# The first pair of an attention kernel: its first load in two halves by head, its scores and maxima head by head

## The chip, the cores and the metric

The kernel runs on one core of a Trainium2 chip. The metric is the device time of one execution in microseconds (us), the median of the runs. TensorE (PE, with its weight loads PEld) multiplies matrices, VectorE (DVE), ScalarE (ACT) and GpSimd (POOL) work on elements, and SyncE (SP) issues transfers. Each engine has its own queue of instructions, taken in order; semaphores order the queues among each other.

## The reference

A block of causal attention with a linear memory, followed by two feed-forward networks, all in float32. 4 batches of 8 heads, 576 positions, 64 values per head:

```python
def _attn_ref(q, k, v, M_prev, z_prev, beta):
    scores = scale * np.matmul(q, k.transpose(0, 1, 3, 2))
    scores = np.where(causal, -1000000000.0, scores)
    scores = scores - scores.max(-1, keepdims=True)
    a = np.exp(scores)
    a /= a.sum(-1, keepdims=True) + 1e-09
    local = np.matmul(a, v)
    q_p = phi(q)                    # phi(x) = max(x, 0) + min(exp(x), 1)
    mem_ret = np.einsum('bhsd,bhde->bhse', q_p, M_prev)
    mem_norm = np.einsum('bhsd,bhd->bhs', q_p, z_prev)[..., None] + 1e-06
    mem_out = mem_ret / mem_norm
    g = 1.0 / (1.0 + np.exp(-beta))[None, :, None, None]
    return g * mem_out + (1 - g) * local
def reference(...):
    x = attention output as 2304 tokens x 512
    x = _moe_ref(x)     # (silu(x @ w_gate) * (x @ w_val)) @ w_out, inner width 1536
    return _moe2_ref(x) # g(x @ w_in) @ w_out with a clipped square g, inner width 2048
```

## The kernel before, in words

The 32 heads are taken two at a time, as 16 pairs. In a pair the 576 rows of queries are cut into tiles: i = 4, 3, 2, 1 of 128 rows each, in this order, and the first 64 rows. Tile i needs width(i) = 64 + 128 i columns of keys because of the causal mask: 576, 448, 320 and 192. In the numbering of the kernel j = 4 p + k is tile 4 - k of pair p, so j = 0 is tile 4 of pair 0, j = 1 its tile 3.

For every tile TensorE makes the scores of both heads (`scores`, line 1390; head 0 lies on partitions 0 to 63 of `qk`, head 1 on 64 to 127, and each writes its own columns of PSUM), VectorE adds the mask, negates, takes the row's extreme and writes `negs` and `nmax` (`tile_max`, line 1067, head by head, each with a readout), ScalarE takes the exponential and its sum (`exp_tile`, 807), VectorE makes the factor of the memory part from that sum and the norms (`mem_scale`, 1086), GpSimd writes the memory's rows beside the exponentials (`mem_rows`, 681), TensorE turns both over (`turn`, 1420), ScalarE and VectorE copy them from PSUM (`copy_pt`, 828 and 1105), and TensorE multiplies with V and the memory (`values`, 1442 and 1447). The scores of the first 64 rows are one product (`scores_f`, 1400).

The norms of a pair go another way. ScalarE takes exp(q) (`exp_q`, 797), GpSimd max(q, 0) (`relu_q`, 654), VectorE joins them (`phi`, 1041), GpSimd multiplies with z in two instructions (`phi_z`, 662 and 664, which write `qz`), VectorE sums (`norm_q`, 1047) and takes the reciprocal with the gate (`rnorm_q`, 1052 and 1055); only then can it make the first `mem_scale` of the pair. GpSimd also scales V by the other gate (`v_scale`, 672).

The start, in the order of each queue. SyncE: the columns of `qk` that tile 4 needs, 704 of 1280, as one transfer of 352 KB (line 579, semaphore `ld_first`), the rows `nat` of pair 0, the rest of `qk`, then `nat` of pair 1, V, and so on. ScalarE: a transfer of `beta`, its exponentials (864), `exp_q(0)`, then for pair 0 `exp_tile(0)`, `exp_q(1)`, the wait for `gone` and two copies of it into `cf` (880, 881), `exp_tile(1)` and the rest. GpSimd: masks, `relu_q(0)`, `phi_z(0)`, then `relu_q(1)`, `mem_rows(0)`. VectorE: the small mask, the gates (1137 to 1144) as soon as ScalarE has the exponentials of beta, `tile_max(0)`, a memset and the reciprocal `gone` (1147, 1148), `phi(0)`, `tile_max(1)`, and then the loop: `norm_q(0)`, `rnorm_q(0)`, `mem_scale(0)`, `tile_max(2)`, `tile_max(3)`, and so on. TensorE: 10 idle products of 128x128 on zeros (`idle_products`, 1366; a product of float32 leaves two records in the trace), the scores of tile 4, 4 idle products, `scores_f(0)`, the scores of tiles 3, 2, 1, 8 idle products, and the first `turn`. `scores_f` and the scores of tile 3 both wait until both maxima of tile 4 have been read out (`maxed` at 2), since they write over their columns: tile 3's head 0 and head 1 take the first two banks, which head 0 of tile 4 held.

After the attention of all pairs the two feed-forward networks run on TensorE (lines 1476 to 1478), each product as three on parts of the numbers.

## Time and profile before

| | before |
|---|---|
| median of 3 runs | 979.85 us (979.78 to 980.0) |
| profiled execution, its own time | 979.51 us |
| its span in the trace | 977.70 us |
| PE busy | 966.3 us (99%) |
| DVE, ACT, POOL busy | 696.6, 463.3, 336.2 us |
| attention, until the first feed-forward product | about 183 us of the span |

The profile counts a TensorE record as busy from its start to a modelled end, so records overlap. "Idle before" in brackets is the time for which the engine had nothing to do ahead of a group, with what ended it. A chain of waits follows the last instruction back to what released it, each time to the instruction that came last. Transfers are timed from issue to landing, and a transfer's landing is counted on 16 engines; the median of them is printed.

### The profile page before, as it was taken

Reading aid. Unit: us, or ns where it says so; the run is one execution under the profiler, and the core shown is the slowest. Engines: PE = TensorE matmul, PEld = TensorE weight load, DVE = VectorE, ACT = ScalarE, POOL = GpSimd, SP = SyncE. Lnnn points to the kernel's source line nnn. Section 1 sums busy time; section 2 is a strip of 40 time slices with the busy share of each in tenths; the row PEclk is TensorE's granted clock in tenths of the full one; section 3 lists DMA queues with packets and bytes.
Section 4 is the critical chain, followed back from the end, with each engine's and each line's share of the span. In section 5 each row is a group of like instructions: output and inputs, shape, how many; then the busy total and the mean of one; then the engine's idle time right before and its main releaser. Section 6 shows DMA issues by size and latency. Waiting matters only on the chain.

```text
span 977.7 us, 18964 instructions
## 1 busy us (share of the span) xinstructions
PE 966.3 (99%) x6372; PEld 926.6 (95%) x6372; DVE 696.6 (71%) x1369; ACT 463.3 (47%) x940; POOL 336.2 (34%) x385
## 2 busy tenths in 40 slices
PE   8999999999999999999999999999999999999998
PEld 7777777899999999999999999999999999999998
DVE  6888989576667555557555568888887677867766
ACT  6899999555445222224222246445543333433331
POOL 5777786196782000100000157688410010000000
PEclk9999999999999999999999999999999999999999
DMA  6544543598777755555554544667785744538321
GB/s 246 170 153 155 160 157 110 199 341 286 288 271 307 246 194 199 220 219 217 219 208 194 195 148 169 229 256 258 297 270 200 275 181 174 216 140 301 139 105 65
DMA packets 46157, 204.73 MB, mean 209 GB/s; under 512 B 5488, under 2 KB 5872, under 8 KB 46064
## 3 DMA queue, kind: packets, MB, share of 16 engines
q1 hardware_dynamic: 45920, 203.52, 57.3%
q8 instruction: 54, 0.88, 0.4%
q14 instruction: 39, 0.32, 0.1%
q10 hardware_dynamic: 144, 0.00, 0.0%
HBM read 147.33 MB, written 56.17 MB: 208 GB/s over the span
## 4 chain that ended last, share of the span: by engine, by line
PE 90%; ACT 4%; issue 2%; POOL 2%; DVE 2%; ACTq 0%; DVEq 0%; POOLq 0%
PE ps L1476 26%; PE ps L1478 25%; PE ps L1477 25%; PE ps L1447 5%; PE ps L1390 5%; ACT pt L828 3%; PE ps L1420 3%; POOL wu_l L704 1%; DVE xt_l L1128 0%; PE ps L1366 0%; DVE negs L1067 0%; ACT xt_h L859 0%; ACT rown L807 0%; PE ps L1400 0%; POOL wu_r L689 0%
## 5 line engine op out<-in xcount | busy, mean ns | idle before, releaser
L1476 PE MATMUL ps<-xt_h,wu_h 128*128 128x384 f32 x840 | 281.3, 335 | 0.5 <-DVE wu_l L1119 0.2
L1478 PE MATMUL ps<-xt_h,wu_l 128*128 128x384 f32 x840 | 280.7, 334 | 0.0
L1477 PE MATMUL ps<-xt_l,wu_h 128*128 128x384 f32 x840 | 280.6, 334 | 0.0
L1476 PE MATMUL ps<-hid_h,wd_h 128*128 128x384 f32 x672 | 225.1, 335 | 1.8 <-DVE xy L1240 0.9
L1478 PE MATMUL ps<-hid_h,wd_l 128*128 128x384 f32 x672 | 224.5, 334 | 0.0
L1477 PE MATMUL ps<-hid_l,wd_h 128*128 128x384 f32 x672 | 224.5, 334 | 0.0
L1243 DVE TENSOR_TENSOR xy<-xy,ps 128x384 f32<-128x384 f32 x288 | 158.2, 550 | 69.1 <-PE ps L1478 68.9
L923 ACT ACTIVATE hid_h<-hid_r 128x768 fp32r<-128x768 f32 x84 | 70.8, 842 | 204.9 <-DVE hid_r L1217 140.8
L1476 PEld LDWEIGHTS ps<-xt_h,wu_h 128*128 128x128 f32 x840 | 157.7, 188 | 2.6 <-issue 0.8
L1477 PEld LDWEIGHTS ps<-xt_l,wu_h 128*128 128x128 f32 x840 | 157.7, 188 | 0.0
L1478 PEld LDWEIGHTS ps<-xt_h,wu_l 128*128 128x128 f32 x840 | 157.7, 188 | 0.0
L1476 PEld LDWEIGHTS ps<-hid_h,wd_h 128*128 128x128 f32 x672 | 126.1, 188 | 3.7 <-DVE hid_l L1221 2.3
L1477 PEld LDWEIGHTS ps<-hid_l,wd_h 128*128 128x128 f32 x672 | 126.2, 188 | 0.0
L1478 PEld LDWEIGHTS ps<-hid_h,wd_l 128*128 128x128 f32 x672 | 126.2, 188 | 0.0
L1221 DVE TENSOR_TENSOR hid_l<-hid_r,hid_h 128x768 fp32r<-128x768 f32 x84 | 87.3, 1039 | 40.7 <-ACT hid_h L923 40.6
L739 POOL TENSOR_TENSOR traw<-xy 128x384 f32<-128x384 f32 x20 | 23.1, 1178 | 239.3 <-PE ps L1478 239.3
L807 ACT ACTIVATE rown<-negs,nmax 128x576 f32<-128x576 f32 (+3 forms) x128 | 77.1, 605 | 12.0 <-DVE nmax L1067 11.9
L704 POOL TENSOR_TENSOR wu_l<-wu_r,wu_h 128x256 fp32r<-128x256 f32 x65 | 55.2, 877 | 59.9 <-ACT wu_h L838 59.8
L908 ACT ACTIVATE u2s<-ps 128x384 f32<-128x384 f32 x60 | 29.5, 491 | 96.5 <-PE ps L1478 96.4
L1198 DVE TENSOR_TENSOR hb<-u2s,ps 128x384 f32<-128x384 f32 x60 | 33.1, 551 | 52.9 <-PE ps L1478 52.9
L1227 DVE SCALAR_TENSOR_TENSOR tmp<-tmp 128x768 f32<-128x768 f32 x48 | 52.2, 1089 | 22.9 <-ACT tmp L938 22.6
L938 ACT ACTIVATE tmp<-hb,nhalf 128x768 f32<-128x768 f32 x48 | 45.1, 939 | 48.3 <-DVE hb L1198 34.5
(87 smaller groups left out, 1321.0 us busy)
## 6 DMA issues: line engine op xcount, KB each, us to landing
wu_l<-kept_ul SPq DMA_DIRECT2D x40, 896.0 KB, 7.5
wu_h<-kept_uh SPq DMA_DIRECT2D x40, 896.0 KB, 5.6
kept_uh<-wu_h SPq DMA_DIRECT2D x20, 896.0 KB, 6.0
kept_ul<-wu_l SPq DMA_DIRECT2D x20, 896.0 KB, 6.9
wd_h<-kept_dh SPq DMA_DIRECT2D x28, 512.0 KB, 3.7
wd_l<-kept_dl SPq DMA_DIRECT2D x28, 512.0 KB, 5.2
wu_r<-w_up SPq DMA_DIRECT2D x20, 512.0 KB, 5.2
qk<-qk_in SPq DMA_DIRECT2D x15, 640.0 KB, 5.2
```

Source lines behind the costliest of these rows:

```text
L704: low = nc.gpsimd.tensor_tensor(wu_l[u % 3][:, k], wu_r[u % 3][:, k], wu_h[u % 2][:, k - 1].bitcast(F32), ALU.subtract)
L807: nc.scalar.activation(head_rows(j)[:, h + (i == 1), D:D + w], negs[:, t % NEGS, 0:w], ACT.Exp, bias=nmax[:, p % 2, k:k + 1], scale=-1.0, ...
L923: nc.scalar.activation(hid_h[:, t % 6], hid_r[:, t % 6], ACT.Copy).then_inc(hh_done, 1)
L938: nc.scalar.activation(tmp[:, r], hb[:, u % 2, r], ACT.Relu, bias=nhalf[:], scale=0.5).then_inc(relued, 1)
L1221: nc.vector.tensor_tensor(hid_l[:, t % 6], hid_r[:, t % 6], hid_h[:, t % 6].bitcast(F32), ALU.subtract).then_inc(hl_done, 1)
L1227: nc.vector.scalar_tensor_tensor(tmp[:, r], tmp[:, r], 1.0, tmp[:, r], ALU.min, ALU.mult).then_inc(s_done, 1)
L1243: nc.vector.tensor_tensor(y, y, o, ALU.add).then_inc(evac, 1)
L1390: mm = nc.tensor.matmul(psf[:, col + a0:col + a1], qk[rows, s, P + q0(i):P + q0(i) + P], qk[rows, s, P + S + a0:P + S + a1], start=True, s ...
L1447: mm = nc.tensor.matmul(ps[D * h:D * h + D, bank, col:col + P], vm[:, s, h, c], pt[:, j % PTS, n], start=(c == 0), stop=(c == i))
L1476: nc.tensor.matmul(dst, w_hi, v_hi, start=start, stop=False, skip_group_check=onto)
L1477: nc.tensor.matmul(dst, w_hi, v_lo, start=False, stop=False, skip_group_check=onto)
L1478: return nc.tensor.matmul(dst, w_lo, v_hi, start=False, stop=stop, skip_group_check=onto)
```

## The change

The first load is issued as two transfers, head 0's 64 partitions on SyncE's queue and head 1's on ScalarE's, ahead of `beta`'s, each with a semaphore of its own. Tile 4 of pair 0 has a function of its own, `scores_first`: it waits for head 0's half, issues both products of head 0, waits for head 1's half, issues those of head 1, and signals each head by itself (`scored_first`, `scored`); `tile_max(0)` waits for the one and then the other. `scores_f` and the scores of tile 3 wait for one maximum of tile 4 and not for two, in every pair (in every pair since that wait is written once for all; tiles 2 and 1 still wait for two). On VectorE `tile_max(0)`, `tile_max(1)` and `phi(0)` come right behind the small mask, in this order, and the gates, the memset and `gone` behind them. On ScalarE `exp_tile(1)` comes ahead of the two copies of `gone`. The idle products of the start go from 10, 4 and 8 to 7, none and 12.

```diff
@@ SyncE
-            sp.dma_start(qk[:, 0, cut:], qk_in[0][:, cut:]).then_inc(ld_first, 16)
+            sp.dma_start(qk[0:D, 0, cut:], qk_in[0][0:D, cut:]).then_inc(ld_first[0], 16)
@@ ScalarE
+            cut = P + q0(SLOTS)
+            act.dma_start(qk[D:P, 0, cut:], qk_in[0][D:P, cut:]).then_inc(ld_first[1], 16)
             act.dma_start(betas[:, 0], beta.rearrange("(o h) -> o h", o=1).broadcast_to([P, 2 * HPB])).then_inc(ld_beta, 16)
...
+                if p < NPAIR:
+                    exp_tile(j + 1)
                 if p == 0:
                     act.wait_ge(gone_set, 1)
...
                 if p < NPAIR:
-                    exp_tile(j + 1)
                     exp_tile(j + 2)
@@ VectorE
-                at_least(dve, scored, j + 2 if i == 2 else j + 1)
+                if j > 0:
+                    at_least(dve, scored, j + 2 if i == 2 else j + 1)
                 for h in range(2):
                     t, k = 2 * j + h, block_of(i, h)
+                    if j == 0:
+                        dve.wait_ge((scored_first, scored)[h], 1)
...
             nc.vector.tensor_copy(maskf[D:P], mask[D:P, S - D:S]).then_inc(maskf_set, 1)
+            dve.wait_ge(maskf_set, 2)
+            tile_max(0)
+            tile_max(1)
+            phi(0)
             dve.wait_ge(gexp_e, 2)
...
-            dve.wait_ge(maskf_set, 2)
-            tile_max(0)
             nc.vector.memset(cf[0:D, :, 0], 1.0).then_inc(cf_set, 1)
             nc.vector.reciprocal(gone[:], gexp[:, 1]).then_inc(gone_set, 1)
-            phi(0)
-            tile_max(1)
@@ TensorE
-            idle_products(10)
+            idle_products(7)
...
-                if j == 0:
-                    pe.wait_ge(ld_first, 16)
-                else:
+                if j > 0:
                     at_least(pe, ld_qk[s], 16 * (p // 2 + 1))
...
-                    at_least(pe, maxed, 2 * SLOTS * p + 2)
+                    at_least(pe, maxed, 2 * SLOTS * p + (1 if i == 3 else 2))
...
+            def scores_first():
+
+                i, w = SLOTS, width(SLOTS)
+                for h in range(2):
+                    rows = slice(D * h, D * h + D)
+                    col = score_col(i, h)
+                    pe.wait_ge(ld_first[h], 16)
+                    for a0, a1 in ((0, 512), (512, w)):
+                        mm = nc.tensor.matmul(psf[:, col + a0:col + a1], qk[rows, 0, P + q0(i):P + q0(i) + P],
+                                              qk[rows, 0, P + S + a0:P + S + a1], start=True, stop=True)
+                    mm.then_inc((scored_first, scored)[h], 1)
...
             def scores_f(p):
...
-                at_least(pe, maxed, 2 * SLOTS * p + 2)
+                at_least(pe, maxed, 2 * SLOTS * p + 1)
...
-                if p < NPAIR:
+                if p == 0:
+                    scores_first()
+                elif p < NPAIR:
                     scores(SLOTS * p)
...
-                if p == 0:
-                    idle_products(4)
...
                     if p == 0:
-                        idle_products(8)
+                        idle_products(12)
                     turn(SLOTS * p, (0, 1))
```

## Rows read from the trace of the kernel before

**Rows 1.** The page, part 4: engines' shares of the chain

```profile
...
PE 90%; ACT 4%; issue 2%; POOL 2%; DVE 2%; ACTq 0%; DVEq 0%; POOLq 0%
...
```

**Rows 2.** Chain of waits in order: start us, length us, what

```profile
...
5.67 1.75 PE ps L1390 x8
...
9.15 0.41 PE ps L1400 x2
...
11.74 0.68 DVE norm L1047
...
18.60 1.23 POOL vm L672
...
19.87 1.31 PE ps L1447 x20
...
30.63 1.28 PE ps L1447 x20
...
```

**Rows 3.** DMA issues before 1 us: count, KB each, us to landing

```profile
...
qk<-qk_in SPq DMA_DIRECT2D x1, 352.0 KB, 4.8
...
```

**Rows 4.** Stretches: busy by engine, granted clock, DMA share, GB/s

```profile
...
2.00:5.00 3.00, 3.00 (x16) 3.00 (x15) 0.45 (x2) 0.44 (x1) 0.21 (x1) 1.00 0.60 135
...
```

**Rows 5.** Weight loads: lines of 2:5 and 11.35:13, timeline of 5.6:6.7

```profile
...
L1366 PEld LDWEIGHTS ps<-pt 128*128 128x128 f32 x15 | 3.3, 333 | 0.0
...
L1366 PEld LDWEIGHTS ps<-pt 128*128 128x128 f32 x16 | 1.9, 191 | 0.2 <-issue 0.2
...
5.62 0.53 PEld L1390 LDWEIGHTS ps<-qk 64*128 64x128 f32 x4 [0.24 <-issue]
6.64 0.20 PEld L1390 LDWEIGHTS ps<-qk 64*128 64x128 f32 x2 [0.49 <-issue]
```

**Rows 6.** Timeline of TensorE: start, length, what, [idle before]

```profile
...
1.03 4.64 PE L1366 MATMUL ps<-pt 128*128 128x128 f32 x20 [1.03 <-DVE pt L1132]
...
7.34 1.16 PE L1366 MATMUL ps<-pt 128*128 128x128 f32 x8
...
9.49 1.89 PE L1390 MATMUL ps<-qk 64*128 64x448 f32 x12
...
14.93 1.30 PE L1390 MATMUL ps<-qk 64*128 64x512 f32 x8
...
```

**Rows 7.** Timeline of VectorE, same columns

```profile
...
6.11 0.19 DVE L1137 TENSOR_SCALAR gexp<-gexp 128x64 f32<-128x64 f32 x1 [3.63 <-ACT gexp L864]
...
7.56 0.76 DVE L1067 CUSTOM_DVE_ANT_0 negs<-ps,mask 128x576 f32<-128x576 f32 x1 [0.70 <-PE ps L1390]
8.25 0.08 DVE L1067 DVE_READ_ACCUMULATOR2_ANT nmax<- 128x1 f32 x1
...
8.93 0.08 DVE L1067 DVE_READ_ACCUMULATOR2_ANT nmax<- 128x1 f32 x1
8.96 0.32 DVE L1148 RECIPROCAL gone<-gexp 128x32 f32<-128x32 f32 x1
...
9.20 0.69 DVE L1041 SCALAR_TENSOR_TENSOR qp<-qexp,qrelu 128x576 f32<-128x576 f32 x1
10.56 0.62 DVE L1067 CUSTOM_DVE_ANT_0 negs<-ps,mask 128x448 f32<-128x448 f32 x1 [0.67 <-PE ps L1390]
...
11.66 0.75 DVE L1047 TENSOR_REDUCE norm<-qz 128x9 f32<-128x576 f32 x1
...
```

**Rows 8.** Timeline of GpSimd, same columns

```profile
...
9.98 0.32 POOL L662 TENSOR_TENSOR qz<-qp,nat 128x64 f32<-128x64 f32 x1 [1.27 <-DVE qp L1041]
10.25 1.28 POOL L664 TENSOR_TENSOR qz<-qp,nat 128x512 f32<-128x512 f32 x1
...
```

**Rows 9.** Timeline of ScalarE, same columns

```profile
...
9.99 0.68 ACT L797 ACTIVATE qexp<-nat 128x576 f32<-128x576 f32 x1
...
11.23 0.67 ACT L807 ACTIVATE rown<-negs,nmax 128x448 f32<-128x448 f32 x1
...
13.71 0.56 ACT L807 ACTIVATE rown<-negs,nmax 128x320 f32<-128x320 f32 x1 [1.07 <-DVE nmax L1067]
...
```

More of the change, by code:

```diff
@@ L153, in attention_two_ffns @@
         r_in = [sem(f"r_in{s}") for s in range(2)]
-        ld_first = sem("ld_first")
+        ld_first = [sem(f"ld_first{h}") for h in range(2)]
+        scored_first = sem("scored_first")
         r_row = sem("r_row")
```

## The prediction

> **What bounds the kernel now.** I read four views. First the page: the chain that ended last is TensorE for nine tenths of the span [rows 1], so almost everywhere the time is set by a queue that the change doesn't touch. Then the chain in order of time, from the start to the second pair [rows 2]. It shows where the change can act: the first scores (ending at 5.67 + 1.75 = 7.42 us), the first maxima, the rest of pair 0's scores from 9.15, VectorE's sum of the norms at 11.74, GpSimd's scaling of V at 18.60, and TensorE's first products with V at 19.87. The same products of the next pair come at 30.63, 10.76 us later, and from 19.87 on the attention part of the chain is TensorE's queue with ScalarE's copies between its pieces, pair after pair. So the first 19.87 us are a lead-in, and whatever it gains or loses is, by this chain, handed to the end one for one. Third, the transfers and TensorE's early rows [rows 3 to 6], which say what sets the first score. Fourth, the engines' timelines from 6 to 14 us [rows 7 to 9], which say how long each step of the lead-in takes and who is waiting.
>
> **The first load.** Today one transfer of 352 KB lands at a median of 4.8 us after its issue at 0.72 [rows 3], that is about 5.5, and the weight load of the first scores starts at 5.62 [rows 5]. The 10 idle products (20 records) fill TensorE from 1.03 to 5.67 [rows 6]. Between 2 and 5 us the DMA engines move only 135 GB/s [rows 4]. The change gives each head 176 KB on its own queue. Bounds for head 0's start S: below, the 7 idle products that are left, 1.03 + 14/20 x 4.64 = 4.28; above, today's 5.65, should the halves share the engines so evenly that the first comes with the last. In the row's terms the 352 KB at 135 GB/s are 2.7 us and half of them 1.3, but the other half runs beside it and the next transfer moves up behind it. I take S = 4.8, nearer to today, for that reason, and head 1 some tenths later; since the two heads use different halves of the array, head 1 overlaps with head 0 as now.
> On this point the Trainium skill (DMA: Bandwidth & Descriptors, Rules for kernel authors) speaks against the change: transfers to two partition halves, from one queue or two, serialize on the same 16 engines and are better left as one. No row of before has two such halves. By that rule S stays at 5.65 and the shift below would be +1.78 (rival B).
>
> **The clock.** The page prints a granted clock of 1.00 from the start, but the rows say otherwise: the weight loads of the idle products take 333 ns each between 2 and 5 us and 191 ns after 11 us [rows 5], the lower and the upper of TensorE's two levels. The first scores straddle the rise: first passes at 5.62 to 5.65, second passes at 6.64 (0.99 us later, with weight loads that are short again) [rows 5], all done at 7.42, so 0.78 after 6.64. A tile of the same shape wholly at the upper level takes 1.30 us [rows 6]. A pass over 512 columns streams as long as four idle records of 128: by the busy time of the weight loads beside them, 4 x 3.3/15 = 0.88 us at the lower level and 4 x 1.9/16 = 0.48 at the upper [rows 5]. If the clock rises when it did, near 6.6, scores that start at 4.8 run: first passes to 5.79, second passes at the lower level to 6.67, and the short rest, 0.78 - 0.48 = 0.30, to about 7.0. So 0.85 us of earlier start buy only 0.42 us: the first maximum starts at 7.14 and not at 7.56 [rows 7].
>
> **From the first maximum to the norms, before and after.** Before: VectorE takes the maxima of both heads of the first tile (7.56, the second read out at 8.93 + 0.08 = 9.01), then runs the reciprocal and phi(0) (9.20, 0.69) while TensorE computes the scores of tile 3, waits 0.67 us for these, takes tile 3's maxima from 10.56, and starts the sum over qz at 11.66 [rows 7]. GpSimd's two products for it ran from 9.98 to 10.25 + 1.28 = 11.53 [rows 8], just hidden by tile 3's maxima. From first maximum to that sum: 11.66 - 7.56 = 4.10 us.
> After: TensorE waits for head 0 alone. Head 0's maximum is read out at 8.25 + 0.08 = 8.33, 0.77 after its start [rows 7]. From a readout to the first-rows product 9.15 - 9.01 = 0.14 [rows 2, 7], from there to tile 3's scores 9.49 - 9.15 = 0.34 [rows 2, 6], from there to tile 3's maxima 10.56 - 9.49 = 1.07: 2.32 us from the first maximum, where VectorE has been free since 9.01 - 7.56 = 1.45. Tile 3's maxima then take 11.66 - 10.56 = 1.10. Only then comes phi(0), which used to lie in the gap: 0.69, then 0.09 to GpSimd, 1.55 for its two products, 0.13 back: **2.32 + 1.10 + 0.69 + 0.09 + 1.55 + 0.13 = 5.88 us, against 4.10: 1.78 us longer.** The 0.87 us gap (2.32 - 1.45) in front of tile 3's maxima is now empty, and the wait for GpSimd behind phi is new. This is the main term: tile 3's maxima come earlier by 0.68 on this clock, but nothing in the chain wants them, while phi(0) is wanted by GpSimd and moves from 9.20 to about 10.6 + 0.1.
> Everything else I cost at nothing, with its cover. The gate block on VectorE (from 6.11 to 7.56 - 0.70 = 6.86, and the reciprocal, 0.32 with a memset beside it [rows 7]: 1.1 us) moves into the new 1.77 us wait for GpSimd; uncovered it would cost 1.1. ScalarE now has exp_q(1) waiting for phi(0), with the exponentials of tile 3 queued behind it, then the two gate copies: from phi's end at 11.26, 0.1 + 0.68 [rows 9], then tile 3's exponentials, today from 11.23 to the start of the idling at 13.71 - 1.07 = 12.64 (1.4), then the gate copies, today between 9.99 + 0.68 and 11.23 (0.6), so about 14.1. The next thing wanted of it is tile 2's exponential, which today starts at 13.71 after 1.07 us of idling [rows 9] and will be wanted at 15.1. About 1 us of cover is left. The load of beta issues one descriptor set later; its users now run four microseconds later. The loads of pair 2 wait for qz and go out later by the shift; their use is a period later than the 14.93 at which pair 1's scores start [rows 6], near 25.6, and a landing took 4.8 us. In the later pairs the softer wait (one maximum for two) changes nothing that the chain shows: there the turns of the pair before stand between tile 4's scores and this wait, and VectorE has 2% of the chain [rows 1]. The idle products moved behind the scores (12 instead of 8) end before the first turn as now, since that waits for GpSimd's row.
>
> **Sum.** Advance of the first maximum -0.42, longer way +1.78: **+1.36 us** at the sum over qz, and from there every engine's order is the same as before, so TensorE's products at 19.87 go to 21.2 and the end with them. The profiled execution takes 979.51 us (span 977.70); it becomes 980.87. The median of the runs lies 0.34 above the profiled one, so 979.85 + 1.36 = 981.2 us.
>
> **Rivals.**
> *A, the clock rises late (slower).* Three idle products fewer leave TensorE empty from 4.28 to 4.8, and the four behind the first scores, which today run from 7.34 for 1.16 us [rows 6], are gone, leaving it empty from about 7.0 to 8.05. If by this the rise comes only after about 8 us, the first scores end at about 7.15 (the 0.30 grows to some 0.5), and the product of first rows and tile 3's scores, 1.39 us, run at the lower level and grow by about 1.0. Shift: -0.28 + 1.78 + 1.0 = +2.5, 982.4; if the first turn is still slow, some 0.8 more, 983.2. For it: today's rise followed 5.6 us of unbroken products. Against: it rose within the first tile, and most of the stretch before stays filled.
> *B, the halves land together.* S = 5.65, no advance: +1.78, 981.6; with head 0 0.3 later still, 982.0. For it: one set of engines at 135 GB/s. Against: nothing runs there before, so that the low rate may be a start-up that two queues pass sooner. This is the case that the rule of the Trainium skill (same page and section) describes.
> *C, early clock.* S = 4.28 and the whole tile at the upper level, 1.30: first maximum at 5.72, an advance of 1.84, against 1.78: nothing gained or lost, 979.8. A rise about 1 us earlier than now gives +0.4 to +0.9. This is also the most that the change can give by its own means.
> *D, the delay is absorbed.* If V's scaling were late for another reason than the norms, the way would not count and only the advance would: 979.4. Against: the chain goes through the sum of norms at 11.74 and GpSimd at 18.60 [rows 2].
>
> **How the numbers follow.** Main case 0.56 (its own range +1.06, S = 4.28 with a late rest, to +1.78: 980.9 to 981.6), A 0.20, B 0.12, C 0.07, D 0.05. The range leaves out D, the lower half of C and the upper part of A: 980.1 to 982.9. A measurement of this kernel can tell about 0.2% from no change, 1.96 us; the line lies at 981.81. Slower: A, four tenths of B, a little of the main case: 0.27. Faster by 0.2% needs an advance that even C doesn't give: 0.01. Same: 0.72.
>
> **What would show it.** After the change: the first weight load of the scores near 4.9, the next pass at 6.6; tile 3's maxima on VectorE near 9.5 with idle time before them released by the scores; phi near 10.6; GpSimd's first qz product near 11.4; the sum over qz near 13.0 with idle time released by GpSimd; first products with V near 21.2, next ones 10.76 later. The prediction is wrong if the sum over qz starts before 12.3 (the first scores came much earlier, or at the upper level), or if weight loads after 7 us still take 333 ns (A), or if the interval from first maximum to the sum isn't near 5.9.

## The result and the profile after

The changed kernel takes 983.67 us (median of 7 runs, 982.37 to 984.49) against 980.00 us for the kernel before beside it (7 runs, 979.77 to 980.74): a ratio of 1.0037, with an interval of 1.0028 to 1.0047. It is slower, by about 3.7 us where 1.4 were forecast, and lies 0.8 us above the range. The profiled execution is the second longest of the seven. The profiled execution took 984.36 us with a span of 982.5 (before: 979.51 and 977.7), so the two traces are 4.8 us apart.

The chain's shares are those of [rows 1] but for a point of VectorE:

```profile
PE 90%; ACT 4%; issue 2%; POOL 2%; DVE 1%; DMA 1%; SPq 0%; ACTq 0%; DVEq 0%; POOLq 0%
```

The new item is DMA with 1%: the chain of the changed kernel begins with a transfer. Its steps in order of time (start, length, what):

```profile
1.97 5.41 DMA qk<-qk_in
...
7.43 0.58 PE ps L1419 x2
8.01 1.82 PE ps L1396 x4
...
11.03 0.67 DVE qp L1046
...
12.18 1.18 DVE gt L1156
...
13.40 0.60 DVE gt L1156
...
14.56 0.62 DVE norm L1052
...
16.60 1.06 PE ps L1439 x8
...
17.70 2.32 PE ps L1396 x8
...
23.71 1.24 PE ps L1466 x20
...
34.40 1.28 PE ps L1466 x20
```

Against [rows 2], the sum of the norms is at 14.56 instead of 11.74 and the first products with V at 23.71 (23.64 in TensorE's timeline) instead of 19.87. The next ones start 10.73 us later in both timelines (at 34.37; before at 30.60). From there the distance between the two traces stays at 3.7 to 3.8 us as far as 640 us: the lead-in hands its delay on one for one, as forecast. A last 0.95 us is added near 650 us (see the end).

The starts in the lead-in, from the timelines of both traces:

| start of, us | before | after | later by |
|---|---|---|---|
| first scores | 5.65 | 4.27 | -1.38 |
| first maximum | 7.56 | 5.72 | -1.84 |
| product of first rows | 9.15 | 7.43 | -1.72 |
| tile 3's maxima | 10.56 | 9.85 | -0.71 |
| phi(0) | 9.20 | 10.94 | +1.74 |
| GpSimd's product for qz ends | 11.53 | 13.33 | +1.80 |
| sum over qz | 11.66 | 14.47 | +2.81 |
| first turn (TensorE) | 13.83 | 16.60 | +2.77 |
| first products with V | 19.87 | 23.64 | +3.77 |

Three engines' timelines tell where it goes (start, length, engine, line, operation, out<-in, count, [idle before and what ended it]). TensorE:

```profile
4.27 2.19 PE L1409 MATMUL ps<-qk 64*128 64x512 f32 x8
7.43 0.58 PE L1419 MATMUL ps<-qk 128*128 128x64 f32 x2 [0.96 <-DMA qk<-qk_in]
7.93 3.38 PE L1396 MATMUL ps<-qk 64*128 64x448 f32 x12
...
16.60 1.06 PE L1439 MATMUL ps<-ident,rown 128*128 128x128 f32 x8 [2.40 <-POOL rown L683]
17.70 2.32 PE L1396 MATMUL ps<-qk 64*128 64x512 f32 x8
```

VectorE:

```profile
9.85 0.62 DVE L1075 CUSTOM_DVE_ANT_0 negs<-ps,mask 128x448 f32<-128x448 f32 x1 [2.58 <-PE ps L1396]
...
10.94 0.76 DVE L1046 SCALAR_TENSOR_TENSOR qp<-qexp,qrelu 128x576 f32<-128x576 f32 x1
...
12.11 1.89 DVE L1156 COPY gt<-gexp 64x16 f32<-64x16 f32 x2
...
14.47 0.70 DVE L1052 TENSOR_REDUCE norm<-qz 128x9 f32<-128x576 f32 x1
```

GpSimd:

```profile
12.06 1.27 POOL L666 TENSOR_TENSOR qz<-qp,nat 128x512 f32<-128x512 f32 x1
13.30 1.64 POOL L656 TENSOR_SCALAR qrelu<-nat 128x576 f32<-128x576 f32 x1
```

The reader is to see five things. Head 0 is scored early. TensorE then stands empty for 0.96 us, until the product of first rows is released by the transfer of the rest of the first pair's q and k. Tile 3's scores take 3.38 us against 1.89 in [rows 6], with 1.92 instead of 1.07 until their maxima can start. Two copies of 64x16 elements take 1.89 us. And the tile after the first turn takes 2.32 us against the 1.30 of [rows 6]. The granted clock says why the scores are slow (stretch; per engine in the order PE, PEld, DVE, ACT, POOL its busy time; clock, where 1.00 is the upper of TensorE's two levels, 2.4 GHz, and 0.50 the lower, 1.2 GHz; DMA share; GB/s):

```profile
7.60:9.50 1.90, 1.90 (x6) 1.06 (x8) 0.00 (x0) 1.11 (x4) 0.03 (x1) 0.50 1.04 423
9.50:11.00 1.50, 1.50 (x10) 1.02 (x6) 1.15 (x5) 0.00 (x0) 0.00 (x0) 0.50 0.78 314
14.00:17.80 3.80, 1.35 (x12) 0.98 (x11) 3.37 (x18) 1.89 (x7) 1.44 (x3) 1.00 0.91 321
17.80:21.20 3.40, 3.40 (x14) 2.38 (x15) 2.99 (x9) 1.95 (x8) 2.97 (x5) 0.50 1.00 407
```

The clock was at its upper level from 4.3 us (the weight loads change from 333 to 190 ns there), fell to the lower one from 7.6 to 11.0, and fell again from 17.8 to 21.2. Ahead of the first fall TensorE was empty from 6.46 to 7.43, ahead of the second for 2.40 us.

Not every execution had both falls. This one has a mean granted clock of 0.997 over its span. Five of the other six have 0.998, as have the traced executions of e4, g1 and g3, each with one fall of 3.1 to 3.5 us, and the last (984.49 us) has 1.0. So in most executions of the changed kernel one fall is likely, and by f1 and g4 below it is the one at the first turn; the first fall, 1.0 us in the split that follows, belongs to this trace.

**The 2.81 us at the sum over qz, split by these rows:** first maximum -1.84; the longer way, as forecast, +1.78; wait for the rest of q and k +0.81 (7.43, where head 0's readout at 6.48 plus the usual 0.14 gives 6.62); lower clock on the product of first rows (0.50 to tile 3's scores, not 0.34) +0.16 and on tile 3's scores (1.92, not 1.07) +0.85; phi to the end of qz +0.06; the gate block +1.01 (14.47 - 13.33 = 1.14 from the end of qz to the sum, where the forecast has 0.13). The parts add up to 2.83. The slow tile of the second pair adds the next 1.0 behind the sum.

### The profile page after: what moved, and what is told of

The parts are those of the page before. It is cut to its first block, busy times and chain, and to the rows that moved or that the text cites. A ratio compares the mean times of both kernels' runs of the same rounds, so it can differ in the third digit from the quotient of the medians.

```text
span 982.5 us, 18953 instructions
## 1 busy us (share of the span) xinstructions
PE 968.9 (99%) x6366; PEld 927.5 (94%) x6366; DVE 698.0 (71%) x1369; ACT 462.9 (47%) x940; POOL 335.3 (34%) x385
## 4 chain that ended last, share of the span: by engine, by line
PE 90%; ACT 4%; issue 2%; POOL 2%; DVE 1%; DMA 1%; SPq 0%; ACTq 0%; DVEq 0%; POOLq 0%
PE ps L1495 26%; PE ps L1496 25%; PE ps L1497 25%; PE ps L1466 5%; PE ps L1396 5%; PE ps L1439 3%; ACT pt L830 3%; DMA qk<-qk_in 1%; POOL wu_l L706 1%; PE ps L1419 0%; ACT wu_h L840 0%; ACT rown L809 0%; POOL wu_r L691 0%; POOL wu_r L689 0%; DVE xy L1251 0%
## 5 line engine op out<-in xcount | busy, mean ns | idle before, releaser
L1075 DVE CUSTOM_DVE_ANT_0 negs<-ps,mask 128x576 f32<-128x576 f32 (+3 forms) x128 | 63.7, 553 | 10.2 <-PE ps L1396 6.9
```

The source lines that it names most:

```text
L1075: nc.vector.tensor_tensor_reduce(negs[:, t % NEGS, 0:w], psf[:, col:col + w], mask[:, S - w:S], -(float(D) ** -0.5), 3.0e38, ALU.add, ALU. ...
```

## The experiments

Fifteen kernels ran, in four groups on one chip each. "Trace" is how much later than before (19.87 us) the first products with V start in the one profiled execution; "median" is the difference of the medians to the kernel before in the same group. The ratio is taken over all executions and is not the quotient of the medians.

| kernel | median us | less before | ratio, 95% interval | trace |
|---|---|---|---|---|
| e1_fill | 983.68 | +4.31 | 1.0049 (1.0030 to 1.0067) | +2.13 |
| e2_phi | 980.84 | +1.47 | 1.0012 (1.0003 to 1.0021) | +0.43 |
| e3_fill_phi | 980.21 | +0.84 | 1.0009 (1.0000 to 1.0019) | +1.74 |
| e4_gates | 981.90 | +2.53 | 1.0025 (1.0015 to 1.0034) | +2.73 |
| f1_order | 984.65 | +5.00 | 1.0049 (1.0034 to 1.0064) | +5.21 |
| f2_load | 982.20 | +2.55 | 1.0025 (1.0015 to 1.0034) | +1.97 |
| f3_idle | 983.19 | +3.54 | 1.0031 (1.0020 to 1.0042) | +3.00 |
| f4_before | 979.37 | -0.28 | 1.0001 (0.9991 to 1.0010) | -0.32 |
| g1_own_idle | 983.69 | +4.32 | 1.0046 (1.0029 to 1.0063) | +3.33 |
| g2_first_7 | 980.26 | +0.89 | 1.0009 (1.0000 to 1.0019) | +0.58 |
| g3_no_middle | 981.02 | +1.65 | 1.0015 (1.0006 to 1.0025) | +1.95 |
| g4_order_fill | 982.81 | +3.44 | 1.0038 (1.0023 to 1.0053) | +2.92 |
| h1_halves | 981.46 | +1.79 | 1.0014 (1.0005 to 1.0023) | -0.01 |
| h2_soft_phi | 980.03 | +0.36 | 1.0001 (0.9992 to 1.0010) | -0.36 |
| h3_best | 979.45 | -0.22 | 1.0000 (0.9991 to 1.0009) | -0.42 |

Trace and median need not agree to better than about 1 us, since the moments at which the clock rises and falls differ from one execution to the next; two rows, e1 and h1, are further apart and are taken up below.

**The changed kernel with its clock held.** The four idle products stand ahead of `scores_f`, as before.

```diff
+                if p == 0:
+                    idle_products(4)
...
-                        idle_products(12)
+                        idle_products(24)
```

> The changed kernel with TensorE kept busy in its two holes: 4 idle products behind the first scores, and 24 instead of 12 before the first turn. Theory (three causes: phi behind tile 3's maxima; the clock falls in the holes; the gate copies and GpSimd's products slow each other): weight loads stay near 190 ns from the rise on, the scores of pair 1's tile 4 take 1.3 us and not 2.3, tile 3's maxima start about 8.9 and not 9.85, the sum over qz starts near 13.5 and not 14.5, first products with V near 21.8 (1.9 later than before), time about 981.9 us. Rival (the clock is all of it): about 980 us, like before. Rival (the clock plays no part): unchanged, 983.7 us.

Measured: 983.68 (982.84 to 986.85). In its trace no fall is left: tile 3's maxima at 9.21, the sum over qz at 13.84, the first turn at 15.96 and the products with V at 22.00 instead of 23.64. So the second fall goes with the hole ahead of the first turn; all four executions have a mean clock of 1.0. The times gained nothing, though the trace did. Two of four runs were 1.5 and 4 us over the other two; 24 idle products at the lower level would themselves block the first turn, as f3 and f2 show below, but no slow execution of e1 was traced.

**phi(0) back in its old place.**

```diff
             tile_max(0)
-            tile_max(1)
             phi(0)
+            tile_max(1)
```

> The changed kernel with phi(0) back between the maxima of tile 4 and those of tile 3, all else as changed. Theory: phi ends near 8.4, GpSimd's two products near 10.1, tile 3's maxima still near 9.85 if the clock falls at 7.6; then the gate copies without a product of GpSimd beside them, 1.1 us instead of 2.9; the sum over qz near 12.1 (0.4 later than before), the hole ahead of the first turn 2.4 us shorter, and time near 980.5 us. Rival (clock alone): 983 us.

Measured: 980.84, so moving one operation undoes 2.2 us of the change's 3.7 (3.67 less 1.47). phi started at 8.23, GpSimd had finished qz at 10.62, the gate block ran from 10.57, its two small copies took 0.38 us together, and the sum over qz started at 12.13. With phi early, qz no longer waits for tile 3's maxima, and what holds the sum is VectorE's own queue: the maxima until 10.57 and the gate block behind them. No fall of the clock is in this trace (980.04 us, the second shortest of ten), though TensorE was empty for 1.15 and for 1.09 us in it; seven of the ten executions have a mean clock of 0.998, so most had one, and this is a reason for a median 1.0 us above the trace.

> The changed kernel with phi(0) back between the maxima and 4 idle products behind the first scores; the 12 before the first turn are left. Theory: tile 3's maxima from 8.9 to 10.0, gate copies to 11.1, the sum over qz at 11.1 (0.6 earlier than before), no fall of the clock, time 979.4 us, equal to before or a little faster. Rival (the split load costs by itself): slower than 980 us.

This is e2 with `idle_products(4)` ahead of `scores_f`. Measured: 980.21. In the profiled execution the clock rose only after 10.7 us, tile 3's maxima came at 11.13 and the V products at 21.61, later than in e2; the median is 0.6 us lower than that of e2, with intervals that overlap. The four products are worth at most that, and a single trace can show the opposite of the median.

**The gate block back ahead of tile 3's maxima.**

```diff
             tile_max(0)
-            tile_max(1)
-            phi(0)
...
+            tile_max(1)
+            phi(0)
```

> The changed kernel with the gate copies, the memset and the reciprocal moved up between the maxima of tile 4 and of tile 3, where VectorE waits 2.6 us; phi(0) stays behind tile 3's maxima. Theory: the gate copies take 0.2 us each again, the sum over qz starts 0.13 us behind GpSimd's second product, near 13.5 and not 14.5, time about 982.7 us (1.0 below the changed kernel). Rival (the gate copies are hidden by the wait for GpSimd, as the prediction had it): unchanged, 983.7 us.

Measured: 981.90, 1.8 us less than the e1 of the same group and 1.1 to 1.2 less, each against its own before, than the changed kernel. VectorE's timeline:

```profile
8.23 0.19 DVE L1147 TENSOR_SCALAR gexp<-gexp 128x64 f32<-128x64 f32 x1
...
8.60 0.38 DVE L1154 COPY gt<-gexp 64x16 f32<-64x16 f32 x2
...
13.38 0.76 DVE L1052 TENSOR_REDUCE norm<-qz 128x9 f32<-128x576 f32 x1 [1.68 <-POOL qz L666]
```

The same two copies take 0.38 us together with GpSimd idle, and 1.89 beside its products. The sum over qz starts 0.04 us after qz is complete (13.34), with 1.68 us of idle time released by GpSimd: the wait that the prediction wanted to hide the block in is there, and a block placed in it runs longer than the wait. This shows the cost of the block's place: 1.1 us (tile 3's maxima start at 9.85 in both traces, and the sum at 13.38 instead of 14.47). It also shows that the 0.13 of the forecast is not the time of the hand-over: in [rows 7] the sum at 11.66 follows straight on VectorE's own work.
The Trainium skill (SBUF — State Buffer, Who interferes with whom) says that a VectorE copy in a two-port mode and GpSimd share a port pair, and that whichever issues first holds it for the whole instruction. The trace agrees for GpSimd's product: the first slow copy (12.18, 1.18) ends at 13.36, within 0.03 us of the end of the product at 13.33. It does not for GpSimd's relu, which runs from 13.30 to 14.94 and holds the second copy for 0.60 us only. In e2 the relu starts at 10.59, ahead of all three copies of the block; the first takes 0.57 us instead of 0.23, and the two small ones their usual time while the relu still runs:

```profile
10.79 0.57 DVE L1152 COPY gt<-gexp 128x128 f32<-128x128 f32 x1
11.28 0.38 DVE L1156 COPY gt<-gexp 64x16 f32<-64x16 f32 x2
```

In both traces the held copy ends 0.7 to 0.8 us after the relu's start. So the measurement limits the rule here. By that rule the prediction could have priced the block at the length of GpSimd's product, an estimate of 1.3 us [rows 8].

**One part of the change alone, on the kernel before.** f1 has only the new order of VectorE and ScalarE, g4 the same with 24 idle products ahead of the first turn; f2 is the changed kernel with VectorE's old order; f3 has only the new numbers of idle products; f4 is the kernel before, unchanged.

VectorE in f1 and g4 (ScalarE's `exp_tile(j + 1)` is moved as in the change):

```diff
+            tile_max(0)
+            tile_max(1)
+            phi(0)
             dve.wait_ge(gexp_e, 2)
...
-            tile_max(0)
...
-            phi(0)
-            tile_max(1)
```

TensorE in g4 besides:

```diff
-                        idle_products(8)
+                        idle_products(24)
```

and in f3:

```diff
-            idle_products(10)
+            idle_products(7)
...
-                if p == 0:
-                    idle_products(4)
...
-                        idle_products(8)
+                        idle_products(12)
```

> The kernel before with the changed order on VectorE alone (maxima of tiles 4 and 3, phi(0), then gates) and its twin on ScalarE; one load, all idle products and waits as before. Theory: tile 3's maxima stay at 10.56, phi 11.7 to 12.4, GpSimd's products to 14.0, the gate copies beside them take over 2 us in place of 0.75, the sum over qz near 15.2 (3.5 later than before), and since the first turn waits 3.5 us longer on 8 idle products the clock falls in part of the executions (1 us more): 983 to 984.3 us. Rival (the clock in the start is all): within 0.5 of before. Rival (gates hidden, no fall): +2.3, 981.7.

> The kernel before with the changed order on VectorE and ScalarE, and 24 idle products ahead of the first turn in place of 8. Against f1_order it takes away the hole alone. Theory: the sum over qz is 3.2 us later than before, as in f1_order, but pair 1's scores take 1.3 us again: about 982.8 us (f1_order: 984.65). Rival (the fall of the clock costs nothing there): 984.6.

Measured: f1 984.65, g4 982.81. In f1 TensorE was empty for 3.95 us ahead of the first turn; the clock fell in this hole and stayed low for 6.8 us:

```profile
16.10:22.90 6.80, 5.95 (x24) 4.51 (x25) 5.27 (x22) 3.55 (x13) 3.94 (x7) 0.50 0.82 326
```

(that is the stretch in the windows; TensorE's timeline is next)

```profile
16.95 1.94 PE L1421 MATMUL ps<-ident,rown 128*128 128x128 f32 x8 [3.95 <-POOL rown L681]
18.82 2.40 PE L1391 MATMUL ps<-qk 64*128 64x512 f32 x8
```

and in g4, where idle products fill the hole:

```profile
10.72 5.62 PE L1367 MATMUL ps<-pt 128*128 128x128 f32 x48
16.74 1.06 PE L1421 MATMUL ps<-ident,rown 128*128 128x128 f32 x8 [0.39 <-POOL rown L681]
17.84 1.30 PE L1391 MATMUL ps<-qk 64*128 64x512 f32 x8
```

So the way through phi is +2.96 us at the sum over qz (14.62) and +2.92 at the V products with no clock lost. From the start of tile 3's maxima (9.97) to the end of qz it is 3.5 us, where before the sum came 1.1 us behind that start: 2.4 for the way and 1.1 for the gate block, less 0.6 by which the maxima began earlier in this execution (9.97, not 10.56). The fall that goes with the hole costs 2.3 us more in the traces and 1.6 in the medians. All four executions of f1 have a mean clock of 0.997 or 0.998, all four of g4 have 1.0: that the filled hole prevents the fall holds in every one. The order is by this the largest single part of the change.

> The changed kernel with VectorE's order of before (gates, tile 4's maxima, memset and reciprocal, phi(0), tile 3's maxima): the load in halves, the scores head by head, the softer waits and the fewer idle products are left. Theory: the gates wait for beta's exponentials (6.6) and hold the first maximum back to about 7.4; tile 3's maxima near 9.9, the sum over qz near 11.6, as before: 979.0 to 980.0 us. Rival (the load in halves costs, by what it pushes back): 981 us and more.

Measured: 982.20. With phi and the gate block in their old places the sum over qz started at 11.80, 0.14 later than before, and the first turn still only at 15.83, because the idle products were in its way. They began at 12.3, behind scores of tile 3 that took 3.57 us: in this execution the clock rose only at 13.7, behind all of pair 0's scores. Their weight loads on TensorE:

```profile
12.29 3.50 PEld L1374 LDWEIGHTS ps<-pt 128*128 128x128 f32 x24 [0.44 <-issue]
```

> The kernel before with only the idle products changed: 7, none and 12 in place of 10, 4 and 8. It prices the holes by themselves. Theory: TensorE is empty from 4.3 to 5.6 and from 7.4 to 9.1; the clock's rise comes later than 6.6 in part of the executions, then the first scores and tile 3's take up to 1.5 us more: median 980 to 981 us with a wider spread than before. Rival (clock indifferent to holes of this size): the same as before within 0.3 us.

Measured: 983.19 (982.14 to 984.60, seven runs), nearly as much as the whole change. Windows and TensorE's timeline:

```profile
8.40:15.10 6.70, 6.09 (x23) 4.38 (x24) 4.69 (x18) 4.43 (x12) 4.01 (x5) 0.50 0.67 234
```

```profile
5.96 1.30 PE L1390 MATMUL ps<-qk 64*128 64x512 f32 x8 [1.57 <-DMA qk<-qk_in]
9.01 0.66 PE L1400 MATMUL ps<-qk 128*128 128x64 f32 x2 [1.75 <-DVE nmax L1067]
9.60 3.57 PE L1390 MATMUL ps<-qk 64*128 64x448 f32 x12
13.10 3.91 PE L1366 MATMUL ps<-pt 128*128 128x128 f32 x24
16.85 1.04 PE L1420 MATMUL ps<-ident,rown 128*128 128x128 f32 x8
```

The clock had risen by the first tile (1.30 us) and fell at 8.4, in the second of two holes, 1.57 and 1.75 us. Tile 3's scores took 3.57 us, and the sum over qz came 0.95 later (12.61). Then the 12 idle products stood before a turn that was ready earlier: 3.02 us late at the turn, 3.00 at the V products. Their 24 records took 3.91 us, since they began 1.8 us later than before and ran at the lower level for the first 2.0; the 48 of g4, all at the upper level, took 5.62, which is 2.8 for 24. Idle products fill a hole only while they are shorter than it, and at the lower level they are twice as long (20 records in 4.64 us [rows 6], 0.23 each, against 0.12 in g4).

> The kernel before, unchanged, as a second trace and a second set of times. It shows how far the moment of the clock's rise (6.6 us in the first trace) and the time move by themselves. All theories: the same time as before within 0.1%; if the rise depends on the execution and not on the kernel it lies anywhere between about 4 and 8 us.

Measured: 979.37, V products at 19.55, 0.32 us earlier than in the first trace, with the rise near 4.0 instead of 6.6 us. This is how far two traces of one kernel differ here.

**Which of the idle products matter.**

g1 is the changed kernel with the old numbers, g2 and g3 are the kernel before with one half of f3's edit each (g2 its first two lines, g3 the rest). g1:

```diff
-            idle_products(7)
+            idle_products(10)
...
+                if p == 0:
+                    idle_products(4)
...
-                        idle_products(12)
+                        idle_products(8)
```

> The changed kernel with the idle products of before: 10, 4 and 8. Theory (the new order costs by itself, and the wait for it ahead of the first turn lets the clock fall once more): first scores from 5.7, tile 3's maxima near 9.7, the sum over qz near 14.2, TensorE empty for some 4 us ahead of the first turn, clock low for part of pair 1: 983 to 984.5 us, not better than the changed kernel. Rival (the fewer idle products are all of the loss): 980 us.

> The kernel before with 7 idle products at the start in place of 10; 4 and 8 are left. It parts the first hole (4.3 to 5.6 us) from the second. Theory: the rise of the clock moves in a part of the executions to behind the first scores, which then take 0.5 to 1 us more: 980.0 to 980.8 us. Rival (only the second hole counts): as before within 0.3.

> The kernel before with 10 idle products at the start, none behind the first scores, 12 ahead of the first turn. It prices the second hole (7.4 to 9.1 us). Theory: the clock, risen or not, is low in tile 3's scores in most executions and stays low into the idle products: 981 to 982.5 us. Rival (only the first hole counts): as before within 0.3.

Measured: 983.69, 980.26 and 981.02. The two halves of f3's edit cost 0.89 and 1.65 us alone and 3.54 together: either hole is mostly survived, both are not. In g2's trace the clock rose only at 9.2 us and the V products were 0.58 late; in g3's it fell from 10.2 to 13.7 and they were 1.95 late. But giving the changed kernel its old idle products back (g1) repaired nothing. Tile 3's maxima came at 9.54, and then TensorE stood empty for 3.94 us before the turn at 16.28, since 8 idle products are too few for the longer way; the clock was low from 16.0 to 19.4. The number of idle products must fit the hole that each order leaves.

**The halves alone, and the best of the parts.** h1 is the kernel before with the first load by heads and the scores head by head, and nothing else. h2 is the kernel before with tile 3 waiting for one head, ScalarE's order of the change, and the edit below. h3 is the changed kernel with beta's load issued first on ScalarE's queue, 8, 4 and 12 idle products, the gate block back ahead of the first maxima, and then `tile_max(0)`, `phi(0)`, `tile_max(1)`, memset, reciprocal. h2:

```diff
             tile_max(0)
-            nc.vector.memset(cf[0:D, :, 0], 1.0)
-            nc.vector.reciprocal(gone[:], gexp[:, 1])
             phi(0)
+            nc.vector.memset(cf[0:D, :, 0], 1.0)
+            nc.vector.reciprocal(gone[:], gexp[:, 1])
             tile_max(1)
```

> The kernel before with the load in halves and tile 4's scores and maxima head by head, and nothing else: idle products 10, 4, 8, waits for both maxima, order on VectorE and ScalarE as before. Theory: the 10 idle products hold the scores to 5.6 as before, beta lands behind ScalarE's half, the gates end near 7.4, the first maximum starts within 0.3 us of before: the same time within 0.1%. Rival (the halves cost by what they push back): over 980.3 us. Rival (halves gain): under 979.1 us.

> The kernel before with two parts of the change that cost nothing by the traces so far: tile 3's scores wait for one maximum, and phi(0) comes right behind tile 4's maxima, memset and reciprocal behind tile 3's. One load, idle products as before. Theory: phi 0.2 us earlier, the sum over qz 0.2 earlier: 979.2, no difference that can be measured. Rival: 0.6 us faster, the advance of tile 3's maxima.

> A version meant to beat both: load in halves with beta's transfer first on ScalarE's queue, gates ahead of the first maximum as before, then tile 4's maxima, phi(0), tile 3's maxima, memset and reciprocal; softer waits; idle products 8, 4 and 12. Theory: first maximum at 6.8, phi at 8.3, tile 3's maxima at 9.1, the sum over qz near 10.8 (0.9 earlier): 978.5 us in executions in which the clock has risen by 7 us, 980 where it rises behind tile 3's scores; median near 979. Rival (the clock decides alone and gains nothing): 980 us and more.

Measured: 981.46, 980.03 and 979.45, with the kernel before at 979.67. h1's profiled execution took 979.62 us and its lead-in is that of before to 0.02 us (sum over qz 11.64, V products 19.86), but that was the fastest of 11; three of the others, 981.49 to 982.88, had a mean granted clock of 0.998 and not 1.0. That the halves expose the lead-in to a fall in those is an inference from that mean; no such execution was traced. It doesn't account for the others, which are up to 981.63 us at a mean clock of 1.0. A late rise would not show in that mean (f2's traced execution has 1.0 with the clock low until 13.7 us), but none was seen for h1: what makes its median 1.8 us longer is open. h2 and h3 start the products with V 0.36 and 0.42 us earlier than before, little more than f4, the kernel before itself, does (0.32), and the medians don't resolve it. In h3's trace the sum over qz starts at 11.23, still behind GpSimd:

```profile
11.23 0.75 DVE L1052 TENSOR_REDUCE norm<-qz 128x9 f32<-128x576 f32 x1 [0.31 <-POOL qz L666]
```

phi had started at 8.80 there, 0.72 us after VectorE was free, because it waits for GpSimd's relu of q. No combination tried beats the kernel before by an amount that can be measured.

## Why the prediction was wrong, and where it was right

In short: the forecast put four things at nothing that cost time in the trace, namely the gate block (1.0 us), the wait for the rest of q and k (0.8), the fall of the clock ahead of the sum (1.0) and the one behind it (1.0). An advance that was 1.4 us larger than forecast hid a part of them.

- **The frame held.** The lead-in passes its delay on one for one, and it is GpSimd behind phi behind tile 3's maxima that sets the sum over qz. The longer way was put at 1.78 us; from first maximum to the sum the trace shows 8.75 us instead of 5.88; without the wait, the two costs of the clock and the gate block (0.81, 0.16, 0.85, 1.01) it is 5.92. e2 and g4 show the mechanism from both sides.
- **The clock: the nearest rival was A (0.20), by another way.** The prediction looked for a late rise. In the trace of the change the rise came early, and the clock fell afterwards; a late rise is in the traces of f2, e3 and g2. The step that failed here is that TensorE's holes cost nothing unless the rise is late. The hole behind the first scores was named, but only as a reason for a late rise; the hole ahead of the first turn was not, though the main case itself makes it longer. In the trace of the change this is 0.16 + 0.85 us before the sum and 1.0 behind it. The second of these is shown by f1 and g4. The first rests on one trace, and the hole ahead of it (0.96 us) is shorter than holes that e2 and h1 survived (1.15 and 1.16 us). The test given for A (weight loads still 333 ns after 7 us) would have pointed to it for the wrong reason: they were short at 5 us and 326 ns on average from 8 to 11.
- **"The idle products end before the first turn as now."** So they do at the upper level. Where the clock is low when they start, 12 of them take 3.5 to 3.9 us in all and become what the first turn waits for (f2, f3, g3). This term was not in the sum; in the profiled execution of the change it didn't bite, and f3 prices it at about 2 us (3.02 at the turn less 0.95 at the sum).
- **The gate block, costed at nothing: the step that failed in every trace of the new order.** It was put into a wait of 1.77 us by its length at a place where GpSimd was idle. In its new place it runs beside the very product that the wait is for, and costs 1.0 (e4: 1.1). The same 1.9 us for its two small copies are in the traces of e1, f1, g1 and g4. The prediction priced the block at 1.1 uncovered and took the cover for safe; that the real cost is also 1.1 is a coincidence, since the block ran 2.9 us there and was covered for the rest.
- **The next wait that comes last.** With head 0's maximum ready at 6.48 the product of first rows waits for the rest of q and k, which landed at 7.38: 0.8 us. The prediction checked the load of beta and of the second pair, not this transfer, which before was issued at 1.63, landed 6.0 us later and was wanted only at 9.15, so 1.5 us to spare. The 0.8 is at the low end: in e2, e4, f2 and g1 the same transfer landed at 8.0 to 8.4.
- **The first maximum.** -1.84 instead of -0.42: S was 4.27, the lower bound, because the half on SP's queue landed 3.4 us after its issue and the idle products were the last to end; and the clock rose by then. This is the advance that rival C had (5.72, to the hundredth), with a chance of 0.07, and in part it is luck: C took the whole tile at 1.30 us, while it took 2.19 and the maximum waited for head 0's part alone. S was 4.86 in e1 and 4.71 in f2, near the 4.8 of the main case. The advance gave back what the longer way cost; what made the kernel slower is in the terms above.
- **Rival B** fell: the halves landed 3.4 and 4.4 us after their issues (DMA issues of after: KB, us to landing, in the fence below), the whole one 4.8 [rows 3]. In e1, f2 and h1 the order is the other way round: ScalarE's half after 3.1 to 3.2 us, SyncE's, which head 0 waits for, after 3.9 to 4.0. The rule of the Trainium skill (DMA: Bandwidth & Descriptors, Rules for kernel authors) is that two such transfers serialize and are not worth making; rival B took from it that they would come together at 4.8 or later. The measurement decides for the latency of the first half. What the earlier half is worth by itself is not shown: h1 gains nothing, but its ten idle products hold the first scores until 5.19 us and its gates the first maximum until 7.16 (f4: 7.21).

```profile
qk<-qk_in SPq DMA_DIRECT2D x1, 288.0 KB, 5.4
qk<-qk_in SPq DMA_DIRECT2D x1, 176.0 KB, 3.4
qk<-qk_in ACTq DMA_DIRECT2D x1, 176.0 KB, 4.4
```

- **The range** left out the upper part of A and had no case in which two of its costs came together. The medians of the parts don't add either: the order alone costs 5.0, the idle products alone 3.5, and the change with both 3.7, by these traces because a fall of the clock is paid once and the halves bring the start forward.

Open: the last 0.95 us. Near 650 us the changed kernel waits for VectorE in the feed-forward part (TensorE's waits by releaser; us, count, mean):

```profile
PEld ps L1495 <- DVE hid_l L1229: 0.9, 1, 0.9
PE ps L1495 <- DVE xy L1251: 0.6, 1, 0.6
```

and a step of VectorE's takes 1.56 us beside a GpSimd instruction, where the like step of before took 0.96. VectorE's timeline of before:

```profile
645.60 0.96 DVE L1227 SCALAR_TENSOR_TENSOR tmp<-tmp 128x768 f32<-128x768 f32 x1 [0.89 <-ACT tmp L938]
```

and of after:

```profile
649.41 1.56 DVE L1235 SCALAR_TENSOR_TENSOR tmp<-tmp 128x768 f32<-128x768 f32 x1 [0.91 <-ACT tmp L943]
```

The same two waits and the step of 1.5 to 1.6 us are in the traces of e1, f3, h2 and h3 and not in those of the other kernels. (e1 and e3 besides wait some 0.6 us longer than before for VectorE's `wu_l`.) So it doesn't go with the change. It may also make the two clusters, near 979.3 and 980.1, into which the times of the kernel before fall; that is not shown. Which alignment of the two engines starts it was not tested. Nor was why e1's slower runs are slow.

## What to carry to other kernels

Before a step is moved into an idle stretch, look at what the engine it shares with does in that stretch: in a wait for a product of GpSimd, two small VectorE copies took 1.89 us here instead of 0.38. When a lead-in is made of small pieces, write down TensorE's holes in the new order next to the old ones; holes of 2.0 to 3.9 us ahead of the first turn cost the lower clock in nearly every execution here (after, e4, f1, g1), shorter ones of 1.0 to 1.8 us in some and not in others, and filler must be re-counted for each hole, by its length at the lower clock too. One trace does not show how often a fall happens: look at the mean clock of every execution. And when the first load is made faster, follow the load that comes next: its landing is the new first wait.

## What the runs showed of the hardware

- The granted clock fell behind holes of 0.96 us and 2.40 us (after), 1.75 us (g3) and 2.02 us (e4), and within holes of 1.75 us (f3) and 3.9 us (f1, g1). It did not fall behind holes of 1.15 and 1.09 us (e2) and 1.16 us (h1), and in e4 it rose between 6.8 and 8.4 us, about a hole of 1.46 us. It stayed low for 3.1 to 3.5 us (after, e4, g1, g3) or 6.7 to 6.8 us (f1, f3); in f1 TensorE was busy for 5.95 of the 6.80 us. What decides between them was not isolated.
- The rise at the start of one and the same kernel came at 6.6 us in one trace and 4.0 in another (before, f4); over all kernels it lay between 4.0 and 13.7 us, and the three latest (g2 9.2, e3 10.7, f2 13.7) are kernels with 7 idle products at the start. The granted clock reads 1.00 until its first recorded change; before that, weight loads of 333 ns show the lower level.
- A VectorE copy of 64x16 elements took 0.17 us alone, 1.18 beside a GpSimd product of two tensors, 0.60 when it followed the start of GpSimd's relu by 0.1 us, and 0.17 again when it followed it by 0.7 us (e2).
- Two halves of 176 KB on two queues landed 3.4 and 4.4 us after their issue (h1: 4.0 and 3.1), one load of 352 KB after 4.8; the 288 KB behind them took 5.4 us instead of 6.0, and the exponentials that use beta started at 6.28 instead of 5.73.
